# Attention in items of 64 time steps of two batches, on quarters of the TensorE array

## What is computed

```python
for t in range(S):
    kt, vt, rt = (k[:, :, t], v[:, :, t], r[:, :, t])
    cur = np.einsum('bhd,bhe->bhde', u[None] * kt, vt)
    y[:, :, t] = np.einsum('bhd,bhde->bhe', rt, state + cur)
    state = w[None, :, :, None] * state + np.einsum('bhd,bhe->bhde', kt, vt)
...
h = x @ w_in
sp = np.where(h > 20.0, h, np.log1p(np.exp(np.minimum(h, 20.0))))
g = h * np.tanh(sp)
return (g @ w_out).astype(np.float32)
```

## Time and profile before

| | us |
|---|---|
| median of 3 runs | 920.34 |
| lowest, highest | 918.75, 920.5 |
| the profiled execution | 920.1 |
| its span | 918.6 |
| PE busy | 896.1 (98%) |
| DVE busy | 482.0 (52%) |
| ACT busy | 371.0 (40%) |
| POOL busy | 209.7 (23%) |

### The profile page before, as it was taken

The page is one execution under the profiler, slowest core; times in us unless marked ns, Lnnn a source line. Parts: engine busy times, 40 slices in busy tenths (PEclk is TensorE's granted clock), DMA queues, the critical chain, the costliest instruction groups (busy, mean ns, idle before and its releaser), DMA issues.

```text
span 918.6 us, 11719 instructions
## 1 busy us (share of the span) xinstructions
PE 896.1 (98%) x4994; PEld 739.0 (80%) x4994; DVE 482.0 (52%) x492; ACT 371.0 (40%) x367; POOL 209.7 (23%) x151
## 2 busy tenths in 40 slices
PE   7769999999999999999999999999999999999998
PEld 7758878888888888878888888888888888888887
DVE  6468847555464654544346555444445445454443
ACT  1176665565654556565588631021121111110111
POOL 4375435433351453220014510000000000000000
PEclk9879999999999999999999999999999999999999
DMA  6344424111220221120122401000001000000000
GB/s 256 100 152 127 137 73 152 57 58 50 92 102 6 98 93 58 50 93 8 71 68 71 154 35 35 0 35 35 1 35 35 5 30 1 34 1 1 35 1 35
DMA packets 19477, 57.00 MB, mean 62 GB/s; under 512 B 2912, under 2 KB 5344, under 8 KB 19424
## 3 DMA queue, kind: packets, MB, share of 16 engines
q1 hardware_dynamic: 15696, 46.41, 15.1%
q10 hardware_dynamic: 3728, 9.83, 2.9%
HBM read 44.44 MB, written 9.44 MB: 59 GB/s over the span
## 4 chain that ended last, share of the span: by engine, by line
PE 92%; ACT 2%; DVE 2%; issue 1%; DMA 1%; POOL 1%; ACTq 0%; SPq 0%; DVEq 0%; POOLq 0%
PE y_ps L614 42%; PE h_ps L563 31%; PE a_ps L563 11%; PE o_ps L547 2%; PE a_ps L521 2%; PE o_ps L556 2%; DMA att<-in_att 1%; PE a_ps L531 1%; ACT mid L737 1%; DVE g_lo L860 1%; ACT mid L738 0%; DVE g_hi L858 0%; DVE win_lo L851 0%; ACT L745 0%; ACT mid L745 0%
## 5 line engine op out<-in xcount | busy, mean ns | idle before, releaser
L563 PE MATMUL h_ps<-x_split,win_hi 128*128 128x512 f32 (+1 forms) x864 | 269.2, 393 | 8.6 <-DVE win_lo L851 3.6
L614 PE MATMUL y_ps<-g_hi,wout_hi 128*128 128x512 f32 x576 | 226.1, 392 | 0.0
L614 PE MATMUL y_ps<-g_hi,wout_lo 128*128 128x512 f32 x576 | 224.3, 389 | 0.0
L614 PE MATMUL y_ps<-g_lo,wout_hi 128*128 128x512 f32 x576 | 224.2, 389 | 0.0
L858 DVE CAST g_hi<-mid 128x1024 fp32r<-128x1024 f32 x96 | 89.8, 936 | 247.5 <-PE y_ps L614 246.3
L563 PEld LDWEIGHTS h_ps<-x_split,win_hi 128*128 128x128 f32 x864 | 162.0, 191 | 44.8 <-DVE win_lo L851 4.1
L563 PE MATMUL h_ps<-x_split,win_lo 128*128 128x512 f32 (+1 forms) x432 | 168.3, 390 | 0.0
L860 DVE TENSOR_TENSOR g_lo<-mid,g_hi 128x1024 fp32r<-128x1024 f32 x96 | 130.5, 1359 | 3.3
L614 PEld LDWEIGHTS y_ps<-g_hi,wout_hi 128*128 128x128 f32 x576 | 108.1, 188 | 24.7 <-issue 1.7
L614 PEld LDWEIGHTS y_ps<-g_hi,wout_lo 128*128 128x128 f32 x576 | 108.1, 188 | 22.5
L614 PEld LDWEIGHTS y_ps<-g_lo,wout_hi 128*128 128x128 f32 x576 | 108.1, 188 | 22.0
(11 more groups left out here) (100 smaller groups left out, 808.3 us busy)
## 6 DMA issues: line engine op xcount, KB each, us to landing
att<-in_att SPq DMA_DIRECT2D x22, 584.0 KB, 4.9
att<-in_att SPq DMA_DIRECT2D x22, 512.0 KB, 3.7
w_raw<-in_w_in SPq DMA_DIRECT2D x16, 384.0 KB, 3.2
w_raw<-in_w_out SPq DMA_DIRECT2D x16, 384.0 KB, 3.2
x_dram<-mid ACTq DMA_DIRECT2D x6, 768.0 KB, 5.3
att<-x_dram SPq DMA_DIRECT2D x6, 768.0 KB, 4.4
out<-mid ACTq DMA_DIRECT2D x5, 768.0 KB, 3.8
x_split<-x_split SPq DMA_DIRECT2D x66, 32.0 KB, 2.0
```

The costliest lines, as they stand in the source:

```text
L563: m = nc.tensor.matmul(ps, a, b_, start=n == 0, stop=n == len(terms) - 1)
L614: m = nc.tensor.matmul(y_ps[:, o, :], a, b_, start=unit == 0 and t == 0 and j == 0, stop=unit == UNITS - 1 and t == 1 and j == 2, skip_gro ...
```

## The change

- An item is now 64 times (C = 64) of two batches (a couple), its 128 token rows being batch beta, time t. Again 24 items, four to a group of 512 tokens. The masked score products thereby cover 64 x 64 and not 128 x 128 per batch and head; the state is updated after every 64 times.
- Every attention matmul uses a quarter of the array: 48 or 64 rows by 64 weight columns, and 64 (keys-times-values 48) streamed columns; 16 of them per piece. They are written in pairs (left and right column half of one row half), and the pairs alternate between the row halves.
- item_main(n) is one visit per item, in every second unit of layer 1, behind first_product: it has state, values and keys-times-values of item n and, between them, the scores of item n + 1. PE waits in it for three semaphores that its own earlier pairs set (bank1_left, extra_left, bank0_left).
- The diagonal goes into the score tile by VectorE's predicated copy with an identity mask (own_scores), and GpSimd's fill is gone; in the fast path release too (x_fixed is set once at the start).
- LAG is 2. ScalarE finishes each unit by itself, with two table loads in each unit.
- In the start, item_main(4) stands between the halves of V = 0 and 1, chunks 4 and 5 are loaded before the second gap fill, and five weight blocks instead of three are split before the loop. k's powers for the natural layout are widened by ScalarE (k_wide) before the transposes.
- y_ps has a fourth bank, where keys-times-values goes (extra_bank); a_ps holds scores and outputs.

The core of the diff:

```diff
-C = 128
+C = 64
 CHUNKS = S // C
+COUPLES = B // 2
+ITEM = 2 * C
...
-LAG = 3
+LAG = 2
...
+def main_at(V):
+
+    group, unit = divmod(V, UNITS)
+    if group < GROUPS - 1 and unit % 2 == 0:
+        return PER * (group + 1) + unit // 2
     return None
...
+            def score_pair(n, hh, p, first=True):
+
+                for beta in range(2):
+                    cols = slice(beta * C, (beta + 1) * C)
+                    m = nc.tensor.matmul(work_banks(n)[side(beta), hh, p * C:(p + 1) * C], kr_T(n)[heads_rows(hh), 0, p, cols],
+                                         kr_T(n)[heads_rows(hh), 1, p, cols], start=first, stop=True,
+                                         skip_group_check=True)
+                return m
...
+            def item_main(n):
+
+
+                kv, after = n < N_KV, n + 1 < N_ITEMS
                 pe.wait_ge(scores_done, n + 1)
...
+                pe.wait_ge(x_done, n)
+                pe.wait_ge(state_done, min(n, N_KV))
+                if kv:
+                    pe.wait_ge(k_done, n + 1)
+                if after:
+                    pe.wait_ge(late_T, n + 1 - PER + 1)
+
+                state_pair(n, 1, 0, 0, first=True)
+                if kv:
+                    kv_pair(n, 1, 0)
+                state_pair(n, 1, 0, 1).then_inc(bank1_left, 1)
...
+                pe.wait_ge(bank1_left, n - PER + 1)
+                if after:
+                    score_pair(n + 1, 0, 2, first=False)
+                    score_pair(n + 1, 1, 0, first=False)
+                    score_pair(n + 1, 0, 3, first=False)
+                    score_pair(n + 1, 1, 1, first=False)
+                state_pair(n, 0, 0, 0, first=not after)
...
+                value_pair(n, 0, 0, 0)
+                state_pair(n, 1, 1, 0)
+                value_pair(n, 0, 0, 1)
+                state_pair(n, 1, 1, 1)
+                value_pair(n, 0, 1, 0)
+                value_pair(n, 1, 0, 0)
+                value_pair(n, 0, 1, 1).then_inc(bank0_left, 1)
+                value_pair(n, 1, 0, 1)
...
             for V in range(2 * ALL + LAG):
                 if 2 <= V < 2 * ALL:
                     first_product(V)
-                attention_task(slot_task(V, 0))
+                if V >= 2:
+                    attention_after(V)
                 if V >= LAG:
                     second_product(V - LAG)
-                attention_task(slot_task(V, 1))
...
+            def attention_after(V):
+                n = main_at(V)
+                if n is not None:
+                    if n + 1 < N_ITEMS:
+                        act.wait_ge(scores_done, n + 2)
+                    split_x_hi(n)
...
+                    attention_after(V)
+                    if V > 0:
+                        for U in (0, 1) if V == 1 else (V,):
+                            act.wait_ge(sig_done, U + 1)
+                            act.activation(T[U % 2], T[U % 2], ACT.Arctan).then_inc(atan_done, 1)
+                            act.wait_ge(atan_done, U + 1)
+                            act.activation(T[U % 2], T[U % 2], ACT.Sin, scale=2.0).then_inc(sin_done, 1)
                         act.preload_act_table(ACT.Sigmoid if V + 1 < ALL else ACT.Exp)
...
+                dve.copy_predicated(scores[n % 2][:, :, :, :].rearrange("p s a t -> p (s a) t"),
+                                    diagonal[:, :].bitcast(u32).unsqueeze(1).to_broadcast([128, H, C]),
+                                    own.unsqueeze(2).to_broadcast([128, H, C])).then_inc(diag_done, 1)
```

The start of PE's queue in the changed kernel:

```diff
+            keep_warm(12)
+            item_scores(0)
+            pe.wait_ge(k_wide_done, 1)
...
+            keep_warm(6)
+            early_main(0)
+            item_scores(1)
             keep_warm(4)
...
+            early_main(1)
+            keep_warm(10)
+            item_scores(2)
+            keep_warm(6)
+            early_main(2)
+            item_scores(3)
             first_product(0, half=0)
...
+            early_main(3)
             first_product(1, half=0)
...
+            item_scores(PER)
             first_product(0, half=1)
+            attention_after(0)
             first_product(1, half=1)
```

More of the change, by code:

```diff
@@ L90, in attention_mlp @@
         att = [sb(f"att{i}", [128, A_COLS]) for i in range(2)]
-        scores_main = sb("scores", [128, 2, PAIRS, C])
+        scores = [sb(f"scores{i}", [128, 2, PAIRS, C]) for i in range(2)]
+        slow_sum = sb("slow_sum", [128, 2, ITEM])
         pow_kr = sb("pow_kr", [128, 2, PAIRS, C])
@@ L131, in score_banks, with wide_state @@
[L131 to L141, removed]
+            return buf(n)[rows, at:at + PAD]
+        def wide_state(n, rows, beta, p):
+            at = (beta * PAIRS + p) * D
+            return state[rows, n % 2, at:at + PAD]
@@ L233, in load_chunk @@
             def load_chunk(n):
-                before = n - 2 if n > 5 else n - 4
-                sp.wait_ge(attn_ps, before + 1)
-                sp.wait_ge(kv_ps, min(before + 1, N_KV))
+                last = n - 2 if n >= PER + 2 else n - PER
+                sp.wait_ge(attn_ps, last + 1)
                 load_T(n)
@@ L510, in scores, with kv_pair, item_scores @@
+            def kv_pair(n, beta, p):
+                for hh in range(2):
+                    m = nc.tensor.matmul(kv_piece(n, beta)[side(hh), p * D:(p + 1) * D],
+                                         wide_head(n, 0, 2 * p + hh, side(beta)), natural(n, 2)[side(beta), 2 * p + hh, :],
+                                         start=n >= PER, stop=True, skip_group_check=True)
+                return m
+            def item_scores(n):
+                if n < PER:
                     pe.wait_ge(early_T, n + 1)
@@ new lines, in early_main @@
+                if n >= COUPLES:
+                    for q in range(2):
+                        state_pair(n, 0, 0, q, first=q == 0)
+                        state_pair(n, 1, 1, q, first=q == 0)
+                for k in range(PAIRS):
+                    value_pair(n, 0, k % 2, k // 2, first=n < COUPLES and k == 0)
+                    value_pair(n, 1, k % 2, k // 2, first=n < COUPLES and k == 0)
+                for p in range(PAIRS):
+                    kv_pair(n, 0, p)
+                    m = kv_pair(n, 1, p)
@@ L768, in _ @@
             dve.memset(r_powT[:, :, HALF:HALF + 1], 1.0).then_inc(power_step, 1)
+            dve.wait_ge(consts, 4)
+            for i in range(2):
+                half = slice(i * PAD, (i + 1) * PAD)
+                dve.tensor_copy(causal[half, :], later[half, half]).then_inc(masks, 1)
+                dve.tensor_copy(diagonal[half, :], ident[half, half]).then_inc(masks, 1)
             dve.wait_ge(pow_in, 16)
```

545 lines of the change are left out of this document (274 added, 271 removed).

## The result

The changed kernel takes 904.71 us (median of 4 runs, 904.08 to 905.43) where the kernel before takes 920.25 on the same chip: a ratio of 0.9835, with a 95% interval from 0.9818 to 0.9852. It is 15.5 us faster; the forecast was 40 us faster (880), in a range from 866 to 915 that holds the time. The gain is some two fifths of the forecast one, and the time is nearer to rival B's 900 than to 880. The profiled execution has a span of 903.7 us.

A forecast was written before the change was run, and what follows sets the result against it. The prediction took PE to bound the kernel (92% of what ended last). It summed 920.1 - 30.2 (visits) - 11 (start) + 1 (y_free) = 880 us, with a range from 866 to 915.

The forecast's parts named there:

- rival B: In layer 1: ScalarE and VectorE become the bound, 0.3 us in each of 47 units, start -5: 900 us; chance 0.11.
- The new visit: Per attention item: one PE visit of 1.86 + 0.42 + 0.2 = 2.5 us; 20 visits give -30.2 us.
- The open cost: In the visit: no row shows four quarters at once; 1.86 us if together, 3.7 one half at a time; 1.86 taken.
- the waits of PE for itself: In the visit: three waits for PE's own earlier matmuls cost 0.2 us a visit, bounds 0 and 0.6.
- Rivals A: In the visit: four quarters don't run at once, 128 passes take 3.6 to 3.7 us, total 914 us; chance 0.14.
- C (7.5): In the visit: each change between row halves costs 0.11 us, a visit 7.5 us, total 986 us; chance 0.04.
- moves no matmul away: 0: Between first_product(V) and second_product(V): LAG 2 leaves enough time for the work between, so it costs 0 us.
- The start, -11: Start-up: shorter chain and earlier gap transfers bring V = 2 near 43 us instead of 50; -11 us, bounds -3 and -17.
- y_free at V = 41, +1: At V = 41: ScalarE's 9.1 us of work exceed the 8.16 after which PE wants y_free; +1 us.
- its own sign: What would show rival B: idle PE with ACT mid as releaser in every unit.
- its 869: Lower bound of the forecast's total in us, from -34 for the visits and -17 for the start.
- its 896: Upper bound of the forecast's total in us, from -22 for the visits and -3 for the start.

The follow-up runs named there:

- experiment 8: Changed kernel with a test of 64 x 64 matmuls on four, two and one quarters behind its last second product: 128 passes on four quarters take 2.02 us.
- Experiment 1: Changed kernel with the splits of w_out blocks 2 to 7 one step earlier and w_in blocks 6 and 7 one step later: 888.39 us.
- experiment 2: The kernel before with LAG 2 instead of 3 and nothing else: 937.62 us.
- experiment 4: Changed kernel with LAG 3, and VectorE's attention work and low weight parts ahead of mish: 884.86 us.
- experiment 6: Changed kernel with the earlier w_out blocks, and SyncE's loop issuing chunk load, then gap fill, then weight blocks: 883.46 us.
- experiment 7: Kernel of experiment 6 with weight blocks 1 and 2 loaded behind the first gap fill: 883.15 us.
- experiment 3: Changed kernel with LAG 3 instead of 2 and nothing else: 1034.1 us.

## Why the prediction was right, and where it was wrong

The mechanism of the visit was forecast rightly. What failed is one term that was put at nothing, LAG 2, and one that was put too high, the start.

**The new visit: right.** Forecast 1.86 + 0.42 + 0.2 = 2.5 us, measured 2.35. The open cost, four quarters at once, came out at the lower end (experiment 8), and the waits of PE for itself cost little: the 2.12 us between the products are 0.10 more than 128 passes took in experiment 8. 20 visits are 47 us where 50 were forecast: some 33 us saved instead of 30.2. Rivals A (3.7 us a visit) and C (7.5) fall. Two column halves of one row half have 128 passes in 3.88 us in experiment 8, 61 ns for a pair with its loads.

**LAG 2 "moves no matmul away: 0": wrong, the step that failed.** I checked LAG 2 for g alone. Of the weights the prediction says only that "Four weight blocks and more are ready before V = 2", and nothing of the blocks of w_out behind them. second_product(j) is now due in V = j + 2. The step for block j of w_out has ScalarE's half at V = j + 1 (for j from 2 on) and VectorE's at V = j + 2, behind mish. With LAG 3 that was a unit of cover; it was exactly the unit that was removed. It costs 16.2 us of waiting and some 6.5 of clock behind it, 22.7 in sum where the prediction had 0. Experiment 1 takes the waits away by the steps alone, experiment 2 brings them about in the old kernel by LAG alone, and experiment 4 agrees. (In time, experiment 1 gains 16.3 of the 22.7, because a wait for the gap transfers takes the place of a part; with that gone too, experiment 6 gains 21.2.) It was to be read in the code and in the rows: the earlier trace rows stand after 185 us, when all weights are split, and the wait is only between 80 and 150. I had looked at the pattern of the middle where it is steady, and at the start up to V = 3, and at nothing between.

**The start, -11: mis-sized, about -5.** V = 2's first product begins at 50.72 us (before 50.16) and not at 43; that of V = 4 at 74.81 (before 78.85), and by then one second product more is done: 4.04 + 4.08 = 8.1 us. But the items 4 and 5 are done by then in both kernels, and their 2 x (4.03 - 2.35) = 3.4 us are in the visits' saving already; the scores of item 6, some 0.5 us, are done too. The start's own gain is thus about 8.1 - 3.4 + 0.5 = 5.2 us, an estimate from these rows. The second half-product began at 41.71 and not at 34 to 35:

```profile
34.12 0.69 PE L542 MATMUL y_ps<-scores,mid 64*64 64x64 f32 x32 [0.72 <-issue]
...
40.65 1.13 PE L529 MATMUL a_ps<-att 48*64 48x64 f32 x32 [2.50 <-DVE state L954]
41.71 0.80 PE L667 MATMUL h_ps<-x_split,win_hi 128*128 128x256 f32 x2
```

Item 3's visit (34.12) stands on PE behind the first half-product, and the stall in item 1's visit came on top; the prediction had walked the other engines' queues and not PE's own. Items 2 and 3 were split at 37.2 instead of 30.5. Behind the split PE waits for VectorE's state updates, which end at 40.5, because item 4's scores stand ahead of the second half-product. The gap transfers, issued from 37.23 to about 39 us with 2.3 to 2.4 us to landing (the page's medians), come in that time too, so they add little.

**y_free at V = 41, +1: right.** The wait is 0.9 us, once in the list of waits. The table loads of ScalarE in every unit (two times 47 loads, 1.28 us each) fit, as forecast: no wait of PE names ScalarE between 150 and 450 us. So rival B falls by its own sign, though the measured 904.7 is close to its 900: that closeness is chance.

**The sum.** 880, less 3 for the better visits, plus 6 for the start and 22.7 for the late blocks is 905.7, against 904.7 measured (905.4 in the profiled execution). A slip in the prediction's bounds is harmless: its 869 leaves out the +1 for y_free that its 896 has. And with the blocks early and the gap transfers ahead of the loads the kernel takes 883.5 (experiment 6), close to the forecast 880. A part of that closeness is luck, since experiment 6 also has a better order of SyncE's transfers, which the forecast didn't have, and a start that gave less than forecast. That kernel is 4.0% faster than the one before and 2.3% faster than the changed one, and is the best found here together with that of experiment 7.

## What to carry to other kernels

When a change makes a product due earlier, list all its operands and the step at which each becomes ready, weights too; a unit of cover that nobody needed in the steady middle can be all there is in the first eight units. When an order is given as "queue" or "lag", walk the ring: who waits for the old buffer, who stands behind that one on its engine, and whether the first engine waits for them. And a wait of PE can cost more than itself: behind the three longest of the six here PE's granted clock was 0.50 for 3 to 5 us, which cost 6.5 us on top of 16.2. Last, when a stall is compared between two kernels, compare its start and its end, and not only its length.

## What the runs showed of the hardware

- Four quarters of the array worked side by side in fp32 (experiment 8): 128 passes of 64 x 64 in 2.02 us, against 3.88 on two column halves and 3.87 for 64 passes on one quarter.
- The products behind PE's waits of 3.5 to 6.0 us ran in part at a granted clock of 0.50 (87.3 to 91.4, 112.9 to 118.1 and 139.3 to 142.6 us) and took 5.96 to 7.07 us for 4.30; those behind waits of 0.6, 1.2 and 1.4 us ran at 1.00 and took 4.37, 4.36 and 4.36. In experiment 3 three waits of 2.63 us each had different outcomes: the clock was 0.50 behind the first (92.8 to 97 us), 1.00 behind the second (117.2 to 121.5) and 0.70 behind the third (145.3 to 151).
- PE stood for 1.2 to 2.7 us in the middle of a piece, with no releaser in the profile, at about 20 us in every variant of the changed kernel. It ended at 20.8 to 21.5 us in seven of them, and at 20.19 in the one in which two weight loads come later (experiment 7). The runs don't settle what it is.
